# Attention with two mixtures of experts: how the softmax's reciprocals reach the attention's output

## The reference

```python
def _attn_ref(q, k, v):                       # (2, 8, 1152, 64) each
    q_pool = q.reshape(B, H, S // 2, 2, D).mean(axis=3)          # 576 queries a head
    scores = scale * np.matmul(q_pool, k.transpose(0, 1, 3, 2))
    attn = np.exp(scores - np.max(scores, axis=-1, keepdims=True))
    attn = attn / (np.sum(attn, axis=-1, keepdims=True) + 1e-09)
    return np.matmul(attn, v)
# x: (1152, 512), the heads side by side
# _moe_ref: 4 experts, every token through each, relu(x @ w1[e]) @ w2[e], weighted by domain probabilities
# _moe2_ref: 8 experts, each token through the one of its largest logit, times its gate weight
```

## Time and profile before

| | us |
|---|---|
| median of 3 runs | 897.13 (896.65 to 897.86) |
| the profiled execution | 895.97 |
| its span, first to last instruction | 894.3 |
| PE busy | 839.8 (94%) |
| DVE busy | 398.5 (45%) |
| ACT busy | 315.7 (35%) |
| POOL busy | 208.4 (23%) |

### The profile page before, as it was taken

One profiled execution on the slowest core, in us unless ns is written; L12 is line 12 of the kernel. 1 busy time (PEld: TensorE's weight loads), 2 busy tenths in 40 slices (PEclk: granted clock), 3 DMA queues, 4 the chain that ended last, 5 costly groups with the idle time before them and its releaser, 6 DMA issues.

```text
span 894.3 us, 13134 instructions
## 1 busy us (share of the span) xinstructions
PE 839.8 (94%) x4716; PEld 717.2 (80%) x4717; DVE 398.5 (45%) x646; ACT 315.7 (35%) x514; POOL 208.4 (23%) x179
## 2 busy tenths in 40 slices
PE   7999999999979999999999999999997089999996
PEld 7787778787858998898989998898986068878885
DVE  3775857676763413321414213321413312696235
ACT  3555656564642412220303112220315012675233
POOL 5845865595321000000000000000000501232012
PEclk9999999999989999999999999999998579999998
DMA  8834334342442202110112002110000531596410
GB/s 203 273 85 121 79 86 114 94 106 67 122 131 95 95 1 95 32 64 1 34 61 94 0 0 94 38 58 1 1 1 0 190 140 47 178 330 235 146 42 19
DMA packets 30105, 79.83 MB, mean 89 GB/s; under 512 B 4007, under 2 KB 4007, under 8 KB 30064
## 3 DMA queue, kind: packets, MB, share of 16 engines
q1 hardware_dynamic: 26944, 69.99, 25.7%
q0 software_dynamic: 2960, 8.68, 3.0%
q10 hardware_dynamic: 160, 0.59, 0.3%
HBM read 69.52 MB, written 10.78 MB: 90 GB/s over the span
## 4 chain that ended last, share of the span: by engine, by line
PE 86%; DMA 3%; DVE 3%; POOL 2%; issue 2%; ACT 2%; SPq 0%; POOLq 0%; DVEq 0%; ACTq 0%
PE L L409 23%; PE L L466 23%; PE ring L385 8%; PE scores L350 8%; PE L L581 8%; PE L L555 7%; PE ring L364 5%; PE scores L373 1%; DMA xr<-sorted_rows 1%; DVE negmax L787 1%; POOL sorted_rows L1132 1%; ACT a L612 1%; PE L L563 1%; DMA rawQ<-in_qT 1%; DMA out<-o,destc 1%
## 5 line engine op out<-in xcount | busy, mean ns | idle before, releaser
L409 PE MATMUL L<-xTh,w1h 128*128 128x384 f32 x384 | 129.7, 338 | 6.1 <-DVE w1l L750 6.1
L409 PE MATMUL L<-xTh,w1l 128*128 128x384 f32 x384 | 129.5, 337 | 0.0
L409 PE MATMUL L<-xTl,w1h 128*128 128x384 f32 x384 | 129.4, 337 | 0.0
L658 ACT ACTIVATE hh<-L 128x384 fp32r<-128x384 f32 x96 | 46.6, 491 | 201.3 <-PE L L409 201.3
L466 PE MATMUL L<-w2h,hh 128*128 128x512 f32 x288 | 114.3, 397 | 0.0
L466 PE MATMUL L<-w2h,hl 128*128 128x512 f32 x288 | 113.8, 395 | 0.0
L466 PE MATMUL L<-w2l,hh 128*128 128x512 f32 x288 | 113.7, 395 | 0.0
L886 DVE SCALAR_TENSOR_TENSOR hl<-L,hh 128x384 fp32r<-128x384 f32 x96 | 52.9, 557 | 123.7 <-ACT hh L658 123.3
L1132 POOL DMA_INDIRECT sorted_rows<-acc,posi x9 | 10.7, 1186 | 414.3 <-DVE posi L976 411.9
L612 ACT ACTIVATE a<-scores,negmax 128x1152 f32<-128x1152 f32 x72 | 87.9, 1221 | 37.2 <-DVE negmax L787 37.2
L787 DVE TENSOR_REDUCE negmax<-scores 128x1 f32<-128x1152 f32 x72 | 97.2, 1350 | 3.2 <-PE scores L350 3.0
(11 more groups left out here) (169 smaller groups left out, 1355.8 us busy)
## 6 DMA issues: line engine op xcount, KB each, us to landing
raw<-in_v SPq DMA_DIRECT2D x48, 512.0 KB, 6.0
raw<-in_w SPq DMA_DIRECT2D x32, 512.0 KB, 5.2
rawK<-in_kT SPq DMA_DIRECT2D x32, 288.0 KB, 4.7
rawQ<-in_qT SPq DMA_DIRECT2D x30, 288.0 KB, 5.9
sorted_rows<-filler SPq DMA_DIRECT2D x19, 257.0 KB, 6.0
V<-in_vr SPq DMA_DIRECT2D x16, 288.0 KB, 3.1
xr<-sorted_rows POOLq DMA_DIRECT2D x15, 257.0 KB, 3.0
rawQ<-in_qT ACTq DMA_DIRECT2D x2, 288.0 KB, 6.5
```

The lines of the kernel that those rows point to most:

```text
L409: last = pe.matmul(L1[i % L1_BANKS][:, 0:CW], w[:, d, wf], x[:, cols], start=(n == 0), stop=(n == 3 * DT - 1))
L658: act.activation(hh[c % 2][:, f, :], L1[i % L1_BANKS][:, 0:CW], ACT.Relu) \
```

## The change

The reciprocals go through DRAM. A table `recip` of 8 x 1152 floats is added. For each pair SP writes `rinv` into one row of it, waits for that transfer, and reads the row back in three transfers that give each of 64 partitions the same row, into a new tile `nb` (128 x 576) that replaces `spread`. PE's 5 transposes of a pair, POOL's two copies and DVE's four multiplications go. POOL multiplies `o` with `nb` in one instruction at the head of `split_x`, and `split_x` now stands first in POOL's iteration. For the last pair DVE does the multiplication. The filler rows now stand behind the last pair's transfers in SP's queue.

```diff
+            def share_rinv(j):
+                sp.wait_ge(S["rinv_ready"], j + 1)
+                sp.dma_start(recip[j].rearrange("(t p) -> p t", p=P), rinv[:].rearrange("p a t -> p (a t)")[:, 0:TPP],
+                             allow_slow_non_contiguous=True).then_inc(S["rinv_out"], 16)
+                sp.wait_ge(S["rinv_out"], 16 * (j + 1))
+                at_least(sp, S["y_ready"], j)
+                sp.dma_start(nb[0:DH, :], recip[j, 0:QS].partition_broadcast(DH)).then_inc(S["nb_in"], 16)
+                sp.dma_start(nb[DH:P, FULL * P:], recip[j, QS:QS + XW].partition_broadcast(DH)).then_inc(S["nb_in"], 16)
+                sp.dma_start(nb[DH:P, 0:FULL * P], recip[j, QS + XW:].partition_broadcast(DH)).then_inc(S["nb_in"], 16)
...
                 if n + 2 < NH:
                     load_kq(n + 2, n % 2)
+                if n % 2 == 0:
+                    share_rinv(n // 2 - 1)
+            share_rinv(PAIRS - 1)
...
-            def spread_rinv(g, chunk):
-
-                for t, c in spread_blocks(g):
-                    if c == chunk:
-                        pe.wait_ge(S["spread_ready"], 2 * (g // TPP))
-                        pe.transpose(spare(g + LEAD, c), spread[:, t * P:(t + 1) * P], ident[:]) \
-                            .then_inc(S["nb_ready"], 1)
...
                     score_part(g + LEAD, range(SC))
-                    spread_rinv(g, 0)
-                    spread_rinv(g, 2)
...
             times_v(PAIRS - 1, 1)
-            pe.wait_ge(S["spread_ready"], 2 * PAIRS)
-            for t in range(FULL):
-                last = pe.transpose(L2[1][:, t * P:(t + 1) * P], spread[:, t * P:(t + 1) * P], ident[:])
-            last.then_inc(S["nb_ready"], N_DONE - 1)
-            pe.transpose(L2[0][:, 0:P], spread[:, FULL * P:], ident[:]).then_inc(S["nb_ready"], 1)
...
                     take_last(g - 1)
-                    if spread_blocks(g - 1):
-                        normalize(g - 1)
...
-            tt_(y[:, full], o[:, full], L2[1][:], ALU.mult).then_inc(S["y_ready"], Y_DONE - 2)
-            tail_of_y(PAIRS - 1, L2[0])
+            dve.wait_ge(S["nb_in"], 48 * PAIRS)
+            dve.wait_ge(S["x_lo"], PAIRS - 1)
+            tt_(y[:], o[:], nb[:], ALU.mult).then_inc(S["y_ready"], 1)
...
-            def spread_pair(j):
...
             def split_x(j):
-                pool.wait_ge(S["y_ready"], Y_DONE * (j + 1))
+                pool.wait_ge(S["o_low"], v_done(j, 1))
+                pool.wait_ge(S["o_high"], v_done(j, 1))
+                pool.wait_ge(S["nb_in"], 48 * (j + 1))
+                at_least(pool, S["x_lo"], j)
+                pool.tensor_tensor(y[:], o[:], nb[:], ALU.mult).then_inc(S["y_ready"], 1)
+                pool.wait_ge(S["y_ready"], j + 1)
...
             for j in range(PAIRS):
                 if j:
-                    spread_pair(j - 1)
+                    split_x(j - 1)
                 if j + 1 < PAIRS:
                     prep_k(2 * j + 2, 0)
                     prep_q(2 * j + 2, 0)
-                if j:
-                    split_x(j - 1)
                 if j + 1 < PAIRS:
                     prep_k(2 * j + 3, 1)
                     prep_q(2 * j + 3, 1)
-            spread_pair(PAIRS - 1)
```

More of the change, by code:

```diff
@@ L29 @@
 V_STEP = (5, TPP)
-N_STEP = {2: ((0, 0), (1, 2)), 3: ((2, 0), (3, 2)), 4: ((FULL, 0),)}
 WARM = 28
-Y_DONE = 4
-N_DONE = sum(len(blocks) for blocks in N_STEP.values())
 SC = 3
@@ L55, with attention_moe_moe_kernel @@
 NEPS = 1e-6
-def attention_moe_moe_kernel(nc, kT, qT, vr, dom, w1, w2, emb, tau, v1, v2, rows, out):
+def attention_moe_moe_kernel(nc, kT, qT, vr, dom, w1, w2, emb, tau, v1, v2, rows, recip, out):
     ctx = ExitStack()
@@ L121, in attention_moe_moe_kernel @@
         totale = sb("totale", [P, TPP + 1], F32, att)
-        spread = sb("spread", [P, (FULL + 1) * P], F32, att)
+        nb = sb("nb", [P, QS], F32, att)
         rinv = sb("rinv", [P, 2, FULL + 1], F32, att)
@@ L247, in last_view @@
             return halved(g % TPP, spare(g + LEAD, 1).rearrange("p (i q) -> p i q", q=P))
-        def spread_blocks(g):
-            j, k = g // TPP, g % TPP
-            return N_STEP[k] if j and k in N_STEP else ()
         names = """consts_in kq_in0 kq_in1 v_in0 v_in1 k_hi k_lo q_sum q_scaled q_hi q_lo s_ready max_ready
-            exp_ready den_ready rinv_ready t_ready0 t_ready1 t_ready2 nb_ready a_out0 a_out1 a_out2 o_ready o_low o_high spread_ready y_ready pads_ready emb_in
+            exp_ready den_ready rinv_ready t_ready0 t_ready1 t_ready2 nb_in a_out0 a_out1 a_out2 o_ready o_low o_high rinv_out y_ready pads_ready emb_in
             x_hi x_lo w1_hi w1_lo w2_hi w2_lo l1_ready h_hi l1_free l2_ready l2_free
@@ L622, in take_o @@
                 if s == 0:
-                    at_least(act, S["y_ready"], Y_DONE * j)
+                    at_least(act, S["y_ready"], j)
                 copy(o[s * DH:(s + 1) * DH, 0:HALF], bank(("V", j, s))[0:DH, 0:HALF]).then_inc(S["o_low"], 1)
@@ L802, in take_o @@
                 if s == 0:
-                    at_least(dve, S["y_ready"], Y_DONE * j)
+                    at_least(dve, S["y_ready"], j)
                 dve.tensor_copy(o[s * DH:(s + 1) * DH, HALF:QS], bank(("V", j, s))[DH:P, 0:HALF]) \
@@ L813, in rinv_pair @@
                     .then_inc(S["rinv_ready"], 1)
[L815 to L840, removed]
             dve.wait_ge(S["kq_in0"], 64)
@@ L870, in _ @@
             take_o(PAIRS - 1, 1)
-            o_complete(PAIRS - 1)
-            dve.wait_ge(S["nb_ready"], N_DONE * PAIRS)
-            full = slice(0, FULL * P)
-            tt_(y[:, full], o[:, full], L2[1][:], ALU.mult).then_inc(S["y_ready"], Y_DONE - 2)
-            tail_of_y(PAIRS - 1, L2[0])
+            dve.wait_ge(S["o_low"], NH)
+            dve.wait_ge(S["o_high"], NH)
+            dve.wait_ge(S["nb_in"], 48 * PAIRS)
+            dve.wait_ge(S["x_lo"], PAIRS - 1)
+            tt_(y[:], o[:], nb[:], ALU.mult).then_inc(S["y_ready"], 1)
             last_cols = slice((PAIRS - 1) * QS, PAIRS * QS)
-            dve.wait_ge(S["y_ready"], Y_DONE * PAIRS)
+            dve.wait_ge(S["y_ready"], PAIRS)
             dve.tensor_copy(xTh[:, last_cols], y[:]).then_inc(S["x_hi"], 1)
@@ L1075, in prep_q @@
                     .then_inc(S["q_lo"], 1)
-            def spread_pair(j):
[L1078 to L1084, removed]
-            def split_x(j):
-                pool.wait_ge(S["y_ready"], Y_DONE * (j + 1))
+            def split_x(j):
+                pool.wait_ge(S["o_low"], v_done(j, 1))
[4 more added lines that the diff above has]
+                pool.wait_ge(S["y_ready"], j + 1)
                 cols = slice(j * QS, (j + 1) * QS)
@@ L1190 @@
     rows = nc.dram_tensor("sorted_rows", ((SLOTS + 2) * P, ROW), F32, kind="Internal").ap()
+    recip = nc.dram_tensor("reciprocals", (PAIRS, TPP * P), F32, kind="Internal").ap()
     out = nc.dram_tensor("out_0", (N, D), F32, kind="ExternalOutput").ap()
-    attention_moe_moe_kernel(nc, *aps, rows, out)
+    attention_moe_moe_kernel(nc, *aps, rows, recip, out)
     r = run_bass_kernel_spmd(nc, [feed], core_ids=[0])
```

## The result

The change made the kernel slower: 923.09 us median of four runs (920.52 to 926.36) against 896.93 us of before, a ratio of 1.030 (95% interval 1.028 to 1.032). The forecast was 893.7 us, with a range up to 899.5.

A forecast was written before the change was run, and what follows sets the result against it. PE, DVE and ACT turning in one loop were taken to bound the attention. Gains of 2.5 + 0.5 + 0.35 = 3.4 us, nothing lost, took the median 897.13 to 893.7 us; range 890.5 to 899.5 us.

The forecast's parts named there:

- the price of the write: SP's write of `rinv` to DRAM: 3.1 us as for V's load, plus 1 us for 72 small pieces per engine.
- The trip outlasts its cover: Rival: POOL waits for `nb` once the trip exceeds 11 us, each further microsecond costing one in 6 pairs; chance 0.17.
- The trip's other legs: The three reads back from DRAM after the write: 0.8 us for issuing two, 3.1 us for the last.
- the stretch: PE's attention steps from the scores of k = 2 to the V product of k = 5: 8.45 us becoming 8.09.
- the loop: PE, DVE and ACT taking turns in the attention: 0.36 us gained in each of seven pairs, 2.5 us together.
- the weight parts: DVE's low parts of the weights at the attention's end: with POOL's copies gone, PE starts 0.35 us earlier.
- the five transposes: PE's transposes between the last V product and the next expert tile: their removal gains 0.5 us.
- DVE's 1.30 us would come out whole: Rival: DVE bounds the attention loop, so 1.30 us is gained in each of 7 pairs, 887.2 us; chance 0.10.
- the loop gives nothing back: Rival: delayed `totale` or another rhythm takes back the 0.36 us; only the end's 0.85 us stay, 896.3 us; chance 0.18.
- the moved fillers: Filler transfers moved from beside the attention to behind the last trip, taking 17 us, to 287 us: no cost.
- POOL's extra 1.4 us: The new multiplication in POOL's `split_x`, priced at 1.5 us: covered, so the added work costs nothing.
- DVE's `totale`: Waits for POOL's running instruction: may take 0.7 us, at worst 1.4; cost nothing, at worst some 0.2 us in six pairs.

The follow-up runs named there:

- the 36-byte version: Changed kernel, but each partition's 9 reciprocals written as one run of 36 bytes, in an order other than the reference's: 893.11 us, ratio 0.997.

## Why the prediction was wrong

**The step that failed** is the price of the write. I put it at 3.1 + 1 = 4.1 us; it landed after 8.7 us. "The time per packet falls at least as fast as the bytes do" was an extrapolation from loads and fillers with 1.9 to 3.2 KB a packet. The base was too high (1.4 to 1.9 us measured for 36-byte runs, not 3.1) and the pieces far too low (some 7 us more than runs, not 1). Pieces that lie apart were priced nearly right; crowded ones were in no row. The upper bound of that step, 7.4 us for the pieces, came out near, by accident: a trip of 14.4 us bounded, 13.6 to 15.0 us measured. I gave the rival that hangs on it a chance of 0.17 and cut the range below it.

**The rival had the place right and the price too low.** "The trip outlasts its cover" named the wait (POOL for `nb`), the work behind it and the threshold, 11 us; the trips of 11.2 us without a stall and 12.5 us with one bracket it closely. By its rule of one microsecond per microsecond the measured trips give (14.2 - 11) x 6 - 3.4 = 15.8 us of loss (14.2 is the mean of the six); measured were 26. The stalls came out a little under the rule, 16.5 us and not 19.2. What it lacked is the clock: in the periods with a stall PE runs at its lower clock for a while, 11.4 us in all. The trace of before had this: after a wait of 6.14 us PE's first matmul took 0.66 us, its first one at full clock 0.42 us. I priced stalls by their length alone.

**The trip's other legs.** The reads landed after 4.0 us, with 3.1 us taken for one and 0.8 us for the issues: 4.5 us from the first issue to POOL's start, against 3.9.

**The gains** were nearly right: 8.09 us for the stretch in six pairs, but 8.5 us in pair 1, so that the loop gave 2.1 us and not 2.5; 0.40 us for the weight parts where I had 0.35; the five transposes gone. With the trip covered they give 2.8 us in the profile and 2.3 to 3.6 us in medians, where I had 3.4. The rival by which DVE's 1.30 us would come out whole is refuted by the same stretch, and the one by which the loop gives nothing back by these medians.

**The rest that was priced at nothing** held: the moved fillers (the versions without stall gain what was forecast with the fillers where the change puts them), POOL's extra 1.4 us (1.42 us measured, covered in the 36-byte version), and DVE's `totale`: it ended with POOL's running instruction, after 0.16 to 0.24 us in pairs 3 to 6 of the changed kernel, but after 0.66 and 1.03 us in pairs 1 and 2, the last beyond the 0.9 us put down; whether that cost anything beside the stalls cannot be told from these rows. The Trainium skill's page "DMA: Bandwidth & Descriptors" (Measured) has its 10.5 ns per packet from a load of 64 packets issued by GpSimd; taking it as a price on each engine, as the estimate of 0.76 us did, was my step and not the page's. That estimate is half of what pieces that lie apart took (1.5 us more than runs) and a ninth of what crowded ones took (7 us more). The same page of the Trainium skill (Specifications) notes that below 512 B the engines read, modify and write, which I had left at the slow end. Size alone does not decide: runs of 12 and 36 bytes and single pieces 64 bytes apart are below it too and landed after 1.4 to 3.1 us. Whether that mechanism makes crowding dear no run here shows.

## What to carry to other kernels

An in-order engine's queue is a path: before an instruction that waits for a transfer is put at its head, work out what stands behind it and how long the trip may be, and if the trip's price is unknown, put the instruction behind the work that does not need it. Here that one move turned +3.0% into -0.3% with a trip that was no shorter. It is no shelter from any trip, as the last pair's 18.7 us showed. When a price is bounded from far apart and one end crosses a threshold that multiplies by the number of rounds, the range must reach over it, and a stall of PE must be priced with the slower matmuls after it.

## What the runs showed of the hardware that was not expected

- 1152 values of 4 bytes written from 128 partitions to DRAM land after 1.4 to 1.9 us as runs of 36 bytes, 3.0 us as single pieces 64 bytes apart, and 8.7 to 9.1 us packed (9.8 to 11.9 us to the next issue where the packed write came second).
- For the same distance of 8 bytes, pieces laid out tile by tile land after 5.0 us, partition by partition after 9.0 us.
- Idle times of 2 to 5 us on PE, the shortest 2.06 us, were mostly followed by matmuls at 1.2 GHz (0.32 us apart in place of 0.175), which in the changed kernel cost 11.4 us on top of 16.5 us of idle time.
